# A causal mask added on the vector engine, in the instruction that takes the row maximum

## What is computed

```python
for e in range(E):                       # E = 4
    q = x @ wq[e]
    k = x @ wk[e]
    v = x @ wv[e]
    scores = scale * (q @ k.transpose(0, 2, 1))
    causal = np.triu(np.ones((S, S), dtype=bool), 1)
    scores = np.where(causal, -1000000000.0, scores)
    scores = scores - scores.max(-1, keepdims=True)
    a = np.exp(scores)
    a /= a.sum(-1, keepdims=True) + 1e-09
    ye = a @ v @ wo[e]
    ...
    out += mask[..., None] * w[:, :, kk:kk + 1] * ye
```

## Time and profile before

| | |
|---|---|
| median of 3 runs | 885.29 us (882.73 to 887.86) |
| the profiled execution | 883.76 us |
| its span | 882.0 us |
| mean granted clock of TensorE | 0.996 of full speed |
| TensorE, matrix products | 849.6 us busy, 96% of the span |
| TensorE, weight loads | 736.9 us, 84% |
| VectorE | 484.8 us, 55% |
| ScalarE | 392.0 us, 44% |
| GpSimd | 166.6 us, 19% |

### The profile page before, as it was taken

How to read it: one execution, slowest core, us unless ns; L and a number is a source line. 1 busy time by engine, 2 the same in 40 slices (tenths; PEclk the granted TensorE clock), 3 DMA queues, 4 the chain that set the end, 5 groups by cost and what they waited for, 6 DMA issues and landing times.

```text
span 882.0 us, 17155 instructions
## 1 busy us (share of the span) xinstructions
PE 849.6 (96%) x6797; PEld 736.9 (84%) x6797; DVE 484.8 (55%) x1257; ACT 392.0 (44%) x939; POOL 166.6 (19%) x205
## 2 busy tenths in 40 slices
PE   6798999999999999999999999999999999999898
PEld 3596798978989798987989789897998879897796
DVE  1558745476444755477443775447644575537740
ACT  0447533465234732465234652347423563246521
POOL 0402134002330033201330022400232002410220
PEclk9989999999999999999999999999999999999999
DMA  9910335003050032300331012500304000100001
GB/s 275 233 21 4 106 108 108 14 1 108 2 113 2 1 109 50 71 1 1 109 70 45 2 31 78 120 1 1 108 13 103 1 1 2 43 25 2 1 1 60
DMA packets 117407, 47.31 MB, mean 54 GB/s; under 512 B 94352, under 2 KB 110736, under 8 KB 117328
## 3 DMA queue, kind: packets, MB, share of 16 engines
q1 hardware_dynamic: 117328, 46.21, 21.0%
HBM read 35.19 MB, written 9.44 MB: 51 GB/s over the span
## 4 chain that ended last, share of the span: by engine, by line
PE 75%; DVE 12%; ACT 8%; SPq 2%; issue 1%; DMA 1%; POOL 0%; ACTq 0%; DVEq 0%
PE w L943 35%; PE t L943 20%; ACT probs L621 5%; PE t L997 4%; PE w L982 3%; PE t L1092 3%; DVE neg_max L739 3%; PE t L1013 3%; DVE probs L760 2%; PE t L1078 2%; PE w L1146 2%; PE t L1100 2%; ACT work L636 1%; DVE yT L871 1%; DVE big L788 1%
## 5 line engine op out<-in xcount | busy, mean ns | idle before, releaser
L943 PE MATMUL t<-big,wqk_s 128*128 128x288 f32 x768 | 112.4, 303 | 2.4 <-DVE big L840 1.7
L943 PE MATMUL w<-wout_s,big 128*128 128x512 f32 x432 | 108.1, 399 | 1.5 <-DVE big L788 0.5
L943 PEld LDWEIGHTS t<-big,wqk_s 128*128 128x128 f32 x768 | 105.4, 192 | 3.4 <-issue 2.3
L943 PE MATMUL w<-wsgT_s,big 128*128 128x288 f32 x768 | 107.7, 296 | 0.0
L943 PEld LDWEIGHTS w<-wsgT_s,big 128*128 128x128 f32 x768 | 104.3, 189 | 0.0
L621 ACT ACTIVATE probs<-w,neg_max 128x64 f32<-128x64 f32 (+4 forms) x160 | 83.0, 526 | 45.4 <-DVE neg_max L739 44.8
L943 PEld LDWEIGHTS w<-wout_s,big 128*128 128x128 f32 x432 | 79.6, 188 | 20.3 <-DVE big L788 3.2
L537 POOL TENSOR_TENSOR var_eps<-bn,eps_t 128x1 f32<-128x1 f32 x40 | 13.1, 328 | 413.3 <-DVE bn L776 412.6
L636 ACT ACTIVATE work<-t 128x384 f32<-128x384 f32 (+3 forms) x160 | 63.1, 450 | 44.8 <-PE t L997 42.7
L997 PE MATMUL t<-ident,probs 128*128 128x128 f32 x480 | 72.5, 282 | 7.1 <-DVE probs L760 6.0
L739 DVE TENSOR_REDUCE neg_max<-w 128x1 f32<-128x64 f32 (+4 forms) x160 | 74.0, 484 | 4.4 <-PE w L982 3.4
(11 more groups left out here) (108 smaller groups left out, 1356.4 us busy)
## 6 DMA issues: line engine op xcount, KB each, us to landing
kin<-in_k_dram SPq DMA_DIRECT2D x8, 1024.0 KB, 6.2
vin<-in_v_dram SPq DMA_DIRECT2D x8, 1024.0 KB, 8.9
out_dram<-work SPq DMA_DIRECT2D x32, 256.0 KB, 2.1
qin<-in_q_dram SPq DMA_DIRECT2D x112, 72.0 KB, 2.4
staged_win<-in_moe_w_in_dram SPq DMA_DIRECT2D x4, 512.0 KB, 5.5
staged<-in_moe_w_sg_dram SPq DMA_DIRECT2D x4, 288.0 KB, 3.9
kin<-in_k_dram SPq DMA_DIRECT2D x8, 128.0 KB, 3.0
vin<-in_v_dram SPq DMA_DIRECT2D x8, 128.0 KB, 7.0
```

Source lines behind the costliest of these rows:

```text
L943: last = nc.tensor.matmul(o, stationary(hs, c), mv(hm, c), start=c == of[0] and p == 0, stop=c == of[-1] and p == len(PASSES) - 1)
```

## The change

The mask products go. VectorE adds the mask while it looks for the maximum, with one call, `tensor_tensor_reduce`: it reads the scores in PSUM and a mask of the same width in SBUF, multiplies the sum by -1, writes this over the scores, and gives the minimum as `neg_max`. The exponential then reads negated, masked scores and has a scale of -1. The mask is now 640 columns wide in fp32, zero but for its last 128 columns, so that a slice that ends at its end fits each width K. To make room for it, the rooms `ms` and `row_eps` are given up (sums are updated in place), `ident_h` goes, and `staged` is shortened to what is used.

```diff
-        ident_h = sb("ident_h", [P, P], BF16)
-        causal = sb("causal", [P, P], BF16)
+        causal = sb("causal", [P, SP], F32)
...
-        staged = sb("staged", [P, FC * D + SP], F32)
+        staged = sb("staged", [P, NT * 512], F32)
...
-            pool.wait_ge(ident_ready, 1)
-            nc.gpsimd.tensor_copy(ident_h[:, :], ident[:, :])
             step(nc.gpsimd.memset(causal[:, :], 0.0))
 
-            nc.gpsimd.affine_select(out=causal[:, :], in_=causal[:, :], compare_op=ALU.is_ge, fill=MASKED,
+            nc.gpsimd.affine_select(out=causal[:, SP - P:SP], in_=causal[:, SP - P:SP], compare_op=ALU.is_ge, fill=MASKED,
                                     base=0, pattern=[[-1, P]], channel_multiplier=1)
...
                             exps = nc.scalar.activation(probs[:, j % 2, a, PAD:PAD + K], ps[slot][:, o:o + K], ACT.Exp,
-                                                        bias=neg_max[:, j, a:a + 1], accum_out=row_sum[:, j, a:a + 1])
+                                                        bias=neg_max[:, j, a:a + 1], scale=-1.0, accum_out=row_sum[:, j, a:a + 1])
...
                 def maximum(n, a):
                     V, slot, o, K = scores_at(n, a)
                     u.wait_full(dve, part, V)
-                    nc.vector.tensor_reduce(neg_max[:, n, a:a + 1], ps[slot][:, o:o + K], AX_X, ALU.max,
-                                            negate=True).then_inc(max_ready, 1)
+                    x = ps[slot][:, o:o + K]
+                    nc.vector.tensor_tensor_reduce(x, x, causal[:, SP - K:SP], -1.0, -MASKED, ALU.add, ALU.min,
+                                                   neg_max[:, n, a:a + 1]).then_inc(max_ready, 1)
...
-                    nc.vector.tensor_scalar(row_eps[:, n, :], row_sum[:, n, :], 1e-9, None, ALU.add).then_inc(row_step, 1)
+                    nc.vector.tensor_scalar(row_sum[:, n, :], row_sum[:, n, :], 1e-9, None, ALU.add).then_inc(row_step, 1)
...
-                        if end:
-
-                            d = min(P, w)
-                            for a in range(2):
-                                V, slot, o, K = scores_at(n, a)
-                                o += before + w
-                                nc.tensor.matmul(ps[slot][:, o - d:o], ident_h[:, :], causal[:, P - d:P],
-                                                 start=True, stop=False, skip_group_check=True)
...
-                                    big2[rows, hm, EP + e, PAD + k0:PAD + k0 + w], start=p == 0 and not end,
+                                    big2[rows, hm, EP + e, PAD + k0:PAD + k0 + w], start=p == 0,
```

More of the change, by code:

```diff
@@ L260, in moe_chain @@
         ss = sb("ss", [P, NT, H], F32)
-        ms = sb("ms", [P, NT, H], F32)
         rms_inv = sb("rms_inv", [P, NT, H], F32)
@@ L264, in moe_chain @@
         row_sum = sb("row_sum", [P, N, 2], F32)
-        row_eps = sb("row_eps", [P, N, 2], F32)
         row_inv = sb("row_inv", [P, N, 2], F32)
@@ L512, in body @@
                         pool.wait_ge(ss_ready, count(part + 1, NT, j + 1))
-                        then(nc.gpsimd.tensor_tensor(ms[:, j, :], ss[:, j, :], eps_t[:, :], ALU.add))
-                        nc.gpsimd.tensor_tensor(rms_inv[:, j, :], ms[:, j, :], neg_half[:, 0:H],
+                        then(nc.gpsimd.tensor_tensor(ss[:, j, :], ss[:, j, :], eps_t[:, :], ALU.add))
+                        nc.gpsimd.tensor_tensor(rms_inv[:, j, :], ss[:, j, :], neg_half[:, 0:H],
                                                 ALU.pow).then_inc(rms_ready, 1)
@@ L755, in scale_probs @@
                     dve.wait_ge(row_step, count(part, 2 * N, 2 * n + 1))
-                    nc.vector.reciprocal(row_inv[:, n, :], row_eps[:, n, :]).then_inc(row_step, 1)
+                    nc.vector.reciprocal(row_inv[:, n, :], row_sum[:, n, :]).then_inc(row_step, 1)
                     dve.wait_ge(row_step, count(part, 2 * N, 2 * n + 2))
```

## The result

The changed kernel takes **878.65 us** (median of 7 runs, 877.99 to 879.35) against 884.41 us for the kernel before (median of its 7 runs, the three shown above among them): a ratio of 0.9934, 95% interval 0.9917 to 0.9951. That is 5.8 us faster, with 4.3 to 7.3 by the interval; 4.3 was forecast. Measured again beside the first experiments, the ratio is 0.9939 (0.9916 to 0.9962).

What follows compares the result with a forecast made beforehand. TensorE was taken to bound steps 0 to 4, ScalarE and VectorE steps 5 to 9. Removed products gain 9.1 us, dearer maxima cost 4.8: -4.3 us, from 885.29 to 881.0 us, range 876 to 889.

Steps and rivals of the forecast that it cites:

- The products, 1.19 us a batch: Gain on TensorE from removing mask product pairs in steps 0 to 4 and 8; 9.1 us in all.
- Step 4: Its pair of 128-column mask products, ahead of the last score products on TensorE, was priced at 0.21 us.
- At step 8 the term: The only mask product pair on the chain in the batch's second half, 0.22 us, because VectorE waits for the scores.
- rival 3: Mask products on TensorE gain only 0.84 us a batch, 6.5 us in all, giving 883.6 us; chance 8%.
- The maximum, 0.60 us a batch: Cost on VectorE: each maximum on the path 0.10 us dearer, six a batch, 4.8 us in all.
- ScalarE's readout: Readout after ScalarE's exponential ends 0.09 us after the activation alone; taken as the price of VectorE's second instruction.
- the six maxima: Maxima on the path per batch: both of steps 5 and 7, the first of steps 8 and 9.
- The cover at the first transposes: Slack between step 0's probabilities being ready and TensorE's transposes, 0.63 us, forecast to shrink to 0.05.
- Half rate: VectorE's first instruction takes 1.04 ns a column more: some 26 us slower, 911 us; chance 14%.
- The dear readout: VectorE's readout waits for the first instruction's end, 0.21 us: up to 3.0 us slower, 888; chance 17%.
- The free readout: VectorE's readout costs nothing or is won back in the first instruction: all 9.1 us stay, 876.2; chance 9%.
- The products worth less: Mask product pairs priced by the chain's ends, 0.84 us a batch: 1.7 us faster, 883.6; chance 8%.

Runs made afterwards that it cites:

- the kernel with both masks: The changed kernel with the mask products put back, so the mask is added twice: 885.53 us, ratio 1.0009 to the kernel before.

## Why the prediction was right

**What bounds the kernel: right.** The split into a part bound by TensorE (steps 0 to 4) and one bound by ScalarE and VectorE in turn (5 to 9) held. The first got 0.63 us shorter and the second 0.03 longer, although half of the products lay there. The experiments divide the second: the products gave 0.18 back there, that of step 8, and the maxima took 0.21.

**The products, 1.19 us a batch: too high by 0.37.** The step that failed is "I price a pair by when the first score product starts after it". The time between two starts is what the pair and the wait beside it take together. When the pair goes, only what nothing else holds is won. For steps 0 to 3 a gap of 0.16 us of the weight loads takes its place: 0.08 and 0.12 us came back, not 0.17 and 0.21. Step 4 came out as priced. At step 8 the term was nearly right (0.22 put, 0.18 measured), but not by its reason: the pair cost TensorE 0.41, and VectorE let 0.18 of it through. I had read "VectorE waits for the scores" off the chain without asking how late VectorE itself would be. The chain's own numbers, which I had kept as rival 3 with 8%, were the better ones: 0.07 and 0.13 in steps 0 to 3, and in sum 0.84 a batch against the 0.82 measured.

**The maximum, 0.60 us a batch: too high by 0.39.** The step that failed is "a maximum costs 0.10 us more on a path", with ScalarE's readout as the model and one price for every place. The first instruction's 0.01 us was right (0.03 at 576 columns). The readout has two prices: 0.01 to 0.02 us with the operand in VectorE's own line, as the next instruction starts together with it; 0.07 us for ScalarE, which waits for its result. I had counted four of the six maxima in VectorE's line (steps 5 and 7) and two with ScalarE waiting (8 and 9), and the chain of the kernel with both masks has the same six. At the two prices that is about 4 x 0.02 + 2 x 0.07 = 0.22 us, and 0.21 was measured.

I had set a page of the Trainium skill against my price ("Vector Engine (DVE) Microarchitecture Reference", section 5.2): some 75 ns an instruction, in a row of instructions on VectorE. In VectorE's own line the readout did not cost that here: rows of the changed kernel show two instructions with one start, and 0.01 us more from maximum to maximum. The 0.07 us that ScalarE waits lies near that figure, but it is another thing than the page speaks of.

**The two errors cancelled**: -0.37 and +0.39. The forecast of 4.3 us was right in size for a wrong division; that it came so close was luck. Of the 2.4 us between the 881.0 forecast and the 878.65 measured, 0.9 is the kernel before itself, whose median was 885.29 in the runs that I started from and 884.41 in all. Eight batches at 0.60 us would make 4.8 us, and the medians differ by 5.8. That lies within the interval (4.3 to 7.3), and what the rest is stays open; the profile of the kernel before also started its second batch 1.1 us later than that of the changed kernel, 0.3 of it already at the first projections (43.47 against 43.19), while the repetition of the changed kernel started it only 0.2 us sooner.

**The cover at the first transposes held**: TensorE comes at 277.07 and the probabilities are ready at 276.17 + 0.54 = 276.71. That leaves 0.36 us, where I had feared 0.05.

**The rivals.** Half rate: no, 493 and 778 ns give the time per column of the plain maximum. The rule of the Trainium skill ("Vector Engine (DVE) Microarchitecture Reference", section 7) is on one form of two-source instruction with two non-bf16 sources in SBUF. It did not extend to this one, with a source in PSUM. The dear readout: no. The free readout: nearly so in VectorE's line, not for ScalarE. The products worth less: yes, nearly to the number (0.84 against 0.82), but beside a cheaper maximum, so the time was not the 883.6 us of that rival.

## What to carry to other kernels

The time between the starts of two instructions is not what the first of them costs: ask what else would hold the second back, and test with that instruction alone removed. A result that an instruction writes in a second step has two prices, one for the engine's own line and one for who waits. And work taken off an engine where it waits gives little until the order of the steps is changed to use the wait. Here that gave 0.46 us a batch on top of 0.60.

## What the runs showed of the hardware

- What two mask products (128 columns; weights of 128 rows and 128 columns) cost TensorE depends on their neighbours: 0.42 us between score products (weights of 64 rows; 2.43 - 2.01 us from transposes to values at step 8), 0.21 behind the values' products (weights of 64 columns), 0.12 behind transposes or projections of their own form, and 0.11 behind another pair of their kind. With 64 columns it was 0.08 behind projections and 0.06 behind their kind.
- VectorE's combined sum and minimum, in place over PSUM with a mask from SBUF, takes 1.04 ns a column between 64 and 576 columns (246 and 778 ns), as the plain maximum does (217 and 751 ns). The record of its readout, 141 ns, starts at 285.72, together with that of the next instruction, and ahead of the first instruction's end at 285.80. It cost 0.01 us from maximum to maximum and 0.07 us for ScalarE.
